# Attention, SoLU layer and experts on one core: gates' chain in two parts, other orders of late rows, query sums and first loads

## The reference

```python
q_pool = q.reshape(B, H, S // 2, 2, D).mean(axis=3)
attn = softmax(q_pool @ k.T / sqrt(D)); x = attn @ v      # to [2304, 512]
h = x @ w_in; solu = h * softmax(h)
x = (solu - mean) / sqrt(var + 1e-6) * g_ln @ w_out
xn = x / (norm(x) + 1e-6); en = emb / (norm(emb) + 1e-6)
logits = xn @ en.T / tau; e = argmax(logits)
gate = softmax(logits)[e]
out = gate * (relu(x @ w1[e]) @ w2[e])
```

## Time and profile before

| | us |
|---|---|
| median of 3 runs | 1046.81 (1045.5 to 1047.55) |
| the profiled execution | 1050.58 |
| its span, first to last instruction | 1048.5 |

### The profile page before, as it was taken

One profiled execution on the slowest core, in us unless ns is written; L12 is line 12 of the kernel. 1 busy time (PEld: TensorE's weight loads), 2 busy tenths in 40 slices (PEclk: granted clock), 3 DMA queues, 4 the chain that ended last, 5 costly groups with the idle time before them and its releaser, 6 DMA issues.

```text
span 1048.5 us, 23488 instructions
## 1 busy us (share of the span) xinstructions
PE 1009.4 (96%) x8143; PEld 716.6 (68%) x8143; DVE 705.3 (67%) x1525; ACT 605.4 (58%) x1356; POOL 386.1 (37%) x438
## 2 busy tenths in 40 slices
PE   8899999999999999989999999988799999999996
PEld 6555555555555555547888888866688888888885
DVE  5778787778887877875599998988746514233111
ACT  5777777878777877754734443363456525333221
POOL 3666555666555564472221222151032111111101
PEclk9999999999999999999999999998899999999999
DMA  4533333333333334125000000054665813311100
GB/s 127 130 89 90 78 82 84 84 75 89 90 80 90 82 74 118 31 83 162 21 21 22 20 31 21 25 189 142 228 213 193 285 51 114 120 42 33 41 22 1
DMA packets 97515, 93.64 MB, mean 89 GB/s; under 512 B 49966, under 2 KB 70446, under 8 KB 97264
## 3 DMA queue, kind: packets, MB, share of 16 engines
q1 hardware_dynamic: 92176, 80.20, 25.7%
q0 software_dynamic: 4000, 11.28, 3.3%
q10 hardware_dynamic: 1216, 0.59, 0.2%
HBM read 74.73 MB, written 11.27 MB: 82 GB/s over the span
## 4 chain that ended last, share of the span: by engine, by line
PE 48%; DVE 2%; issue 1%; ACT 1%; POOL 1%; DMA 1%; DVEq 0%; ACTq 0%; POOLq 0%
PE h_ps L770 9%; PE h_ps L772 9%; PE h_ps L771 9%; PE o_ps L770 5%; PE o_ps L772 5%; PE o_ps L771 5%; PE t_ps L1252 2%; PE t_ps L1142 1%; PE h_ps L1219 1%; DVE junk L1353 1%; DMA w_raw_e<-in_moe_w 1%; PE h_ps L1269 1%; ACT w_split L1752 0%; DVE w_split L1571 0%; PE h_ps L1164 0%
## 5 line engine op out<-in xcount | busy, mean ns | idle before, releaser
L375 POOL TENSOR_SCALAR probs<-probs,raises,recips 128x576 f32<-128x576 f32 x272 | 219.9, 823 | 144.7 <-DVE recips L615 144.7
L588 DVE TENSOR_REDUCE lows<-s_ps 128x1 f32<-128x576 f32 x288 | 205.0, 751 | 73.5 <-PE s_ps L499 71.5
L710 ACT ACTIVATE probs<-s_ps,lows 128x576 f32<-128x576 f32 x272 | 199.0, 736 | 86.6 <-DVE lows L588 85.7
L499 PE MATMUL s_ps<-kt,qt 64*128 64x288 f32 x1024 | 162.3, 433 | 3.2 <-ACT probs L710 1.5
L499 PEld LDWEIGHTS s_ps<-kt,qt 64*128 64x128 f32 x1024 | 87.7, 187 | 106.0 <-ACT probs L710 85.5
L538 PE MATMUL pv_ps<-pt,values 128*64 128x512 f32 x576 | 155.2, 617 | 0.3 <-DVE x_t L637 0.2
L1070 POOL DMA_INDIRECT out<-junk,target_rows x25 | 29.8, 1192 | 261.3 <-ACT junk L1792 261.0
L453 PE MATMUL t_ps<-ident,probs 64*128 64x64 f32 x2178 | 118.6, 226 | 6.8 <-ACT pt L705 4.9
L453 PEld LDWEIGHTS t_ps<-ident,probs 64*128 64x128 f32 x2178 | 107.2, 140 | 20.0 <-DVE pt L622 15.7
L622 DVE COPY pt<-t_ps 128x512 f32<-128x512 f32 x144 | 98.8, 686 | 8.1 <-PE t_ps L453 7.4
L1620 DVE TENSOR_TENSOR y_lo<-t_ps,y_hi 128x512 fp32r<-128x512 f32 x50 | 32.4, 685 | 94.7 <-ACT y_hi L1785 94.7
(11 more groups left out here) (280 smaller groups left out, 2093.5 us busy)
## 6 DMA issues: line engine op xcount, KB each, us to landing
w_raw_e<-in_moe_w SPq DMA_DIRECT2D x60, 512.0 KB, 5.3
k_raw<-in_k SPq DMA_DIRECT2D x32, 256.0 KB, 2.7
q_raw<-in_q SPq DMA_DIRECT2D x30, 256.0 KB, 3.9
qt<-qx SPq DMA_DIRECT2D x60, 128.0 KB, 2.4
token_rows<-x_rows SPq DMA_DIRECT2D x18, 256.0 KB, 2.0
values<-in_v SPq DMA_DIRECT2D x32, 128.0 KB, 2.7
values<-in_v SPq DMA_DIRECT2D x64, 64.0 KB, 2.6
w_raw<-in_moe_w_in SPq DMA_DIRECT2D x4, 512.0 KB, 6.6
```

What stands on the lines that cost most here:

```text
L375: nc.gpsimd.tensor_scalar(where, where, raises[:, par, s, c:c + 1], recips[:, par, s:s + 1], ALU.mult, ALU.mult).then_inc(norm_done if c e ...
L499: last = nc.tensor.matmul(s_ps[c][:, u, 0:part], qt[par][rows(u), s, :], kt[par][rows(u), int(s > full), columns(c)], start=True, stop=True)
L588: nc.vector.tensor_reduce(lows[:, g % 2, s, c:c + 1], s_ps[c][:, :, 0:part], AX.XY, ALU.max, negate=True).then_inc(low_done[c], 1)
L710: nc.scalar.activation(two_halves(probs(g, s)[:])[:, :, columns(c)], s_ps[c][:, :, 0:part], ACT.Exp, bias=lows[:, g % 2, s, c:c + 1], scal ...
```

## The change

VectorE's `weigh` becomes two functions: `shift_logits` (up to the shifted logits) stands where low_first(1) stood, after the steps that give the places of tokens; the rest, still called `weigh`, stands before the loop over tiles, after `split_next(1, ...)`. ScalarE's Exp between them moves from tile 2 to just after `split_next(0, ...)`. low_first(0) moves behind tokens_picked, before low_x(0); low_first(1) behind low_x(1). In tile 1, VectorE and ScalarE do the hidden rows (low_h, high_h) and expert 1's second weights before expert 2's first weights. ScalarE takes the last rows after two of the four weight copies, and copies the turned rows itself (it was VectorE). TensorE does late_dot(1) before the 16 matmuls of the first ids. GpSimd adds the queries of pair g + 2 between the second and third batch of pair g, for every pair; the queries Q and the TAILS of pair 2 are turned in slots 1 and 2 instead of 2 and 3. At the start the second keys are loaded once the first have landed (SP waits), and the second queries once the first have (ScalarE waits).

```diff
--- before.py
+++ after.py
@@ -56,9 +56,8 @@
     FIRST_QA, FIRST_QB = range(4, 6)
-    kq_slots = [{0: KA, 1: Q, 2: TAILS, 7: KB} for at in range(pairs)]
-    kq_slots[0] = {4: KA, 5: Q, 6: TAILS, 7: KB}
-    kq_slots[1] = {0: KA, 2: Q, 3: TAILS, 7: KB}
+    kq_slots = {0: KA, 1: Q, 2: TAILS, 7: KB}
+    first_kq_slots = {4: KA, 5: Q, 6: TAILS, 7: KB}
     rest_slots = (4, 5, 6)
@@ -176,11 +175,11 @@
-            return at + 1 < pairs and s in kq_slots[at]
+            return s in (kq_slots if at else first_kq_slots) and at + 1 < pairs
...
-            return kq_slots[at][s]
+            return (kq_slots if at else first_kq_slots)[s]
@@ -202,7 +201,7 @@
-            return len(kq_slots[0]) * (n - 1) + piece + 1
+            return len(kq_slots) * (n - 1) + piece + 1
@@ -283,6 +282,7 @@
             load_k_tail(0)
+            sp.wait_ge(k_in[0], 16)
             load_b(0)
@@ -380,14 +380,13 @@
             for g in range(pairs):
-                if 1 <= g < pairs - 2:
+                normalise(g, 0)
+                normalise(g, 1)
+                if g + 2 < pairs:
                     add_queries(g + 2)
                     add_tail(g + 2)
-                for b in range(len(batches)):
-                    normalise(g, b)
-                if g == 0:
-                    add_queries(2)
-                    add_tail(2)
+                normalise(g, 2)
+                normalise(g, 3)
             pool.wait_ge(t_done[1], key_tiles * (pairs - 1))
@@ -718,6 +717,7 @@
                 act.dma_start(q_tail[rows(h), :], q_heads[h, main:queries, :]).then_inc(q_tail_in, 16)
+            act.wait_ge(q_in[0], 16)
             load_first_q(1)
@@ -1188,13 +1188,13 @@
             turn_rows(1)
+            late_dot(1)
             for m in range(late):
...
                 nc.tensor.matmul(id_first_ps, row_pick[:, m, :], token_first[:, m, :], start=(m == 0), stop=False)
-            late_dot(1)
             pe.wait_ge(hot_first_ready, 1)
@@ -1479,11 +1479,6 @@
                                     ALU.subtract).then_inc(spots_ready, 1)
-            dve.wait_ge(rows_turned, 2)
-            nc.vector.tensor_copy(x_turned_rows[:, 1, :], turned_rows_ps[1]).then_inc(rows_turned_out, 1)
-
-
-            low_first(0)
             dve.wait_ge(late_dots, 2)
@@ -1533,11 +1528,42 @@
+            def shift_logits():
+
+                dve.wait_ge(powered, 1)
+                refine(inv, inv2, squares)
+                then(nc.vector.tensor_tensor(norms, squares[:, tiles:], inv[:, tiles:], ALU.mult))
+                then(nc.vector.tensor_tensor(norms, norms, inv[:, 0:tiles], ALU.mult))
+                then(nc.vector.tensor_scalar(norms, norms, 1e-6, None, ALU.add))
+                then(nc.vector.reciprocal(norms, norms))
+                then(nc.vector.tensor_tensor(norms, norms, inv[:, 0:tiles], ALU.mult))
+                across = [P, tiles, experts]
+                then(nc.vector.tensor_tensor(work[:], lg[:], row[:].unsqueeze(2).broadcast_to(across), ALU.subtract))
+                nc.vector.tensor_tensor(work[:], work[:], norms.unsqueeze(2).broadcast_to(across),
+                                        ALU.mult).then_inc(shifted, 1)
+
+            def weigh():
+
+                dve.wait_ge(exped, 1)
+                then(nc.vector.tensor_reduce(gates, work[:], AX.X, ALU.add))
+                then(nc.vector.tensor_scalar(gates, gates, 1e-9, None, ALU.add))
+                then(nc.vector.reciprocal(gates, gates))
+                then(nc.vector.tensor_tensor(gates, gates, inv[:, 0:tiles], ALU.mult))
+                then(nc.vector.tensor_copy(gate_parts[:, :, 0], gates))
+                then(nc.vector.tensor_tensor(rest, gates, gate_parts[:, :, 0], ALU.subtract))
+                then(nc.vector.tensor_copy(gate_parts[:, :, 1], rest))
+                then(nc.vector.tensor_tensor(gate_parts[:, :, 2], rest, gate_parts[:, :, 1], ALU.subtract))
+                for i in range(3):
+                    done = nc.vector.tensor_tensor(factor_pick[:, :, :, i], tile_pick[:],
+                                                   gate_parts[:, :, i].unsqueeze(2).broadcast_to(wide), ALU.mult)
+                done.then_inc(factors_picked, 1)
+
             def low_x(t):
...
+            low_first(0)
             low_x(0)
@@ -1565,7 +1591,7 @@
-            low_first(1)
+            shift_logits()
@@ -1587,33 +1613,6 @@
-            def weigh():
...
             def low_h(t):
@@ -1621,6 +1620,7 @@
             low_x(1)
+            low_first(1)
             low_h(0)
@@ -1629,15 +1629,17 @@
             split_next(1, 0, w1_hi_done, w1_lo_done)
+            weigh()
             for t in range(1, slot_tiles):
-                if t == 2:
-                    weigh()
                 if t + 1 < slot_tiles:
                     low_x(t + 1)
+                if t == 1:
+                    low_h(t)
+                    split_next(0, part, w2_hi_done, w2_lo_done)
+                if t + 1 < slot_tiles:
                     split_next(t + 1, 0, w1_hi_done, w1_lo_done)
-                low_h(t)
-                if t == 1:
-                    split_next(0, part, w2_hi_done, w2_lo_done)
+                if t > 1:
+                    low_h(t)
                 if t == 2:
@@ -1733,11 +1735,14 @@
             for c in range(part):
+                if c == part // 2:
+                    rows(last)
+                    act.wait_ge(rows_turned, 2)
+                    nc.scalar.copy(x_turned_rows[:, 1, :], turned_rows_ps[1]).then_inc(rows_turned_out, 1)
+                    square_rows(last)
                 act.wait_ge(first_raw_in[part + c], 16)
...
                 nc.scalar.activation(w_split[:, hi:hi + chunk], w_raw[:, part + c, :], ACT.Copy).then_inc(first_w2_hi, 1)
-            rows(last)
-            square_rows(last)
             act.wait_ge(padded, 1)
@@ -1797,23 +1802,25 @@
             split_next(0, 0, w1_hi_done, up_e_done, 0)
+            act.wait_ge(shifted, 1)
+            nc.scalar.activation(work[:], work[:], ACT.Exp).then_inc(exped, 1)
             act.wait_ge(tiles_known, 1)
...
             for t in range(1, slot_tiles):
-                if t == 2:
-                    act.wait_ge(shifted, 1)
-                    nc.scalar.activation(work[:], work[:], ACT.Exp).then_inc(exped, 1)
                 relu(t)
...
                     high_x(t + 1)
+                if t == 1:
+                    high_h(t)
+                    split_next(0, part, w2_hi_done, down_e_done, 0)
+                if t + 1 < slot_tiles:
                     split_next(t + 1, 0, w1_hi_done, up_e_done, halves * (t + 1))
...
                     scale(t - 1)
-                high_h(t)
+                if t > 1:
+                    high_h(t)
                 if t == slot_tiles - 1:
                     scale(t - 1)
-                if t == 1:
-                    split_next(0, part, w2_hi_done, down_e_done, 0)
                 if t == 2:
```

24 lines of the change are left out of this document (removed).

## The result

The changed kernel takes **1040.0 us** (median of six runs, 1038.74 to 1042.85), the kernel before 1046.7 us beside it (six runs, 1045.5 to 1047.55). The ratio is 0.994, with a 95% interval from 0.9927 to 0.9954: 6.3 us less by the ratio, 6.7 us by the medians. Forecast were 10.9 us. The time lies within the range (1033.0 to 1042.0) but outside the band of 1034 to 1036.9 that had the chance 0.54; some 4 us of the gain are missing.

A forecast was written before the change was run, and what follows sets the result against it. TensorE, busy for 96% of the span, was taken as the bound, with only idle time and 1.2 GHz time to win. 7.1 + 2.2 + 1.6 = 10.9 us off 1046.8 gave 1035.9 us, range 1033.0 to 1042.0.

The forecast's parts named there:

- Gates: Experts, tile 2: splitting VectorE's gates chain removes TensorE's 5.43 us wait and the slow clock behind it; 7.1 us won.
- new stall: Before tile 2's products in the experts: low_x(2) starts later behind the moved chain, so TensorE loses 1.17 us.
- term for the clock: Experts, behind the wait for factor_pick: the 5.8 us stretch at 1.2 GHz goes, taken as 2.8 us won.
- Hand-over: SoLU layer to experts: the row maximum comes 2.5 us sooner, 0.3 us is paid; 2.2 us won, bounds 0.7 and 2.5.
- Second pair: Second pair of heads: earlier query sums and turn slots, without the low clock, win 1.6 us; bounds 0.5 and 2.1.
- Rival 1: Second pair of heads: the clock drops as before, costing 1.1 us, so 1037.0 us; chance 0.18.
- Other pairs: 13 more pairs: GpSimd's sums move to slot 8 at price 0; upper bound 0.45 us a pair, lower -0.3.
- Rival 2: Slot 8 of 13 pairs: GpSimd's additions hold VectorE, TensorE waits 0.45 us each; 5.9 us, 1041.8 us; chance 0.11.
- rival 4: Slots 8 and 0 of 13 pairs: VectorE held at both, 18.2 us lost, so slower at 1054.1 us; chance 0.03.
- First loads: Kernel start: first keys and queries loaded alone win nothing; price 0, between -0.3 and +0.5 us.

The follow-up runs named there:

- after: The changed kernel in its first set of runs, against the kernel before: 1040.0 us, ratio 0.9940.
- e10: The changed kernel with GpSimd's query sum done twice in each pair but the first two: 1048.96 us, 1.0017 of the kernel before.
- before: The kernel without the change, the reference of all ratios: 1046.7 us.
- e2: The kernel before with only GpSimd's new order of sums and normalisations and the second pair's new turn slots: 1046.54 us, 0.9996 of the kernel before.
- e4: The kernel before with only the gates part (VectorE's chain split and moved ahead, with ScalarE's Exp): 1040.16 us, 0.9936 of the kernel before.
- e9: The kernel before with only the hand-over part (late rows, their copy, late_dot, low_first(0)): 1045.62 us, 0.9978 of the kernel before.
- e8: The changed kernel without the two waits that keep the first loads alone: 1038.27 us, 0.9915 of the kernel before.
- after_again: The changed kernel itself, run once more beside the others on the same chip: 1039.27 us, 0.9932 of the kernel before.

## Why the prediction was right and wrong, point by point

**Gates, forecast -7.1: right in the mechanism, 1.3 us too large by the marks.** The wait went, the clock stayed up, factor_pick was early, and ScalarE's copies and SP's loads were in time, as priced. The new stall was given as 1.17 us and measured as 1.17 (13.66 less 12.49). In the profiled pair the stretch G is 6.63 us shorter. Over the three kernels with the old chain G is 33.96, 32.69 and 32.89, a mean of 33.2 against 27.4: the term is 5.8 us in the mean. The difference is the term for the clock. The wait for factor_pick was 5.43, 5.12 and 5.75 us in these three; what is left of the longer turn of tile 3 to that of tile 4 (21.46, 20.19 and 20.40 us against 13.7) is 2.3, 1.4 and 0.9 us for the low clock, 1.5 in the mean. I took 2.8 us, half of a stretch of 5.8, from the one execution that I had, and it was the dearest of three.

**Hand-over, forecast -2.2: right.** In the profiled pair it was 1.24 us at tile 0, which lay within the bounds (0.7), for the reason given there: the fill ran to 713.80 at half rate, 6.75 us instead of 5.64. Over ten kernels with it and 16 matmuls and three without, the turn of tile 0 comes 234.60 against 236.86 us after attention, 2.3 us sooner, the turn of tile 1 1.9 us sooner (242.71 against 244.64), and the part alone took 2.2 us off the median. Some of that is the clock's: in two of the ten (after, e10) and two of the three (before, e2) it is low for 10.2 us here, in the others for 6.8 us or less, and at a like clock the turn of tile 1 is 1.3 to 1.6 us sooner.

**Second pair, forecast -1.6: wrong in sign.** The step that failed stands behind this sentence: "the sum starts when the second batch ends, at 31.1 (...), and is there before slot 1 ends". The sum did so, and the wait for q_sum did go; what the new place costs VectorE in the second pair I put at nothing, without a reason. I moved a GpSimd addition of 1.27 us with one of 0.45 right behind it to beside VectorE's two-input steps of slot 8, and asked what that costs only for the *other* pairs. And there I sized it by the rows at hand, 0.63 us (I wrote 0.62) for a step beside GpSimd's normalisations. These are instructions of 0.8 us each; the additions are longer and follow without a gap, and the step was held through both: 2.34 us. In the second pair VectorE's chain to the probs is what TensorE waits for (it waited 0.58 us for them in the kernel before too), so all of it showed: 2.34 less 0.67 us at `weighted` is 2.25 less 0.58 us at TensorE. The measured term is +1.0 us where the clock stays up in both, and 1.7 to 2.0 where it falls in both. The bound should have been taken from the duration of GpSimd's own instruction. The gain that I had hoped for from the clock was one execution's too: e4 and e9 have the old order and no fall there, so the most to be had from the clock was 0.9 us, and not always.

The Trainium skill (SBUF — State Buffer, section "SBUF: two separate sides") says that VectorE's steps with two inputs in SBUF and GpSimd's instructions that read SBUF exclude each other, each for a whole instruction. The traces agree on the holding, and go further in its length: `weighted` was held from 30.44 over the end of one instruction and the whole of two more, and let go at 32.78. In e10, where a gap of 0.18 us stood between the additions, it was out in the gap. Why it slipped in between q_sum and tail_sum in one case (`low` in e10 ended at 33.69, when q_sum did) and not in the other is not settled.

**Rule of the clock.** In the changed kernel the clock fell at 34.55 us, inside TensorE's wait of 2.25 us for the probs (to 35.03) and before the transposes of the queries (37.25). So the rule of the Trainium skill that the forecast weighed here (TensorE: Matmul & The Clock Gate, "PE-mode transpose": a transpose doesn't count as a busy TensorE) was not put to the test, and no run of this study shows more on it than the start of the trace does. The six executions of the new order have the same transposes there, and the clock fell in two of them. Rival 1, a fall as before, is what these two show, though behind a wait that was longer than before.

**Other pairs, forecast 0: right, with the cover named, though not its thickness.** `weighted` 128x4 went from 149 ns to

```profile
L607 DVE TENSOR_TENSOR weighted<-raises,sums 128x4 f32<-128x4 f32 x13 | 11.8, 909 | 0.0
```

and TensorE's waits for the pt copy stayed at 4.9 us. Rival 2 had the mechanism and the wrong place: the slot 8 of the first pair, not the thirteen others. Doubling the sum showed that 1.27 us more is too much for the cover (0.6 us a pair): the mechanism of rival 4 at slot 8, at about half its price.

**First loads, forecast 0: right**, as far as e8 can tell 1 us.

**Together.** The sum by the marks of all profiled executions is -5.8 (gates) - 1.9 (hand-over) + 1.0 (second pair), so -6.7 us, and the measurement is -6.7. The 4.2 us between forecast and measurement are then 2.6 (second pair), 1.3 (gates, the clock) and 0.3 (hand-over). That the sum meets the measurement to the tenth is luck: it leaves out the falls of the clock in the second pair and the 0.6 us of the later pairs, and after_again gave 7.5 us by the medians. The single parts, timed by themselves, add up to -9.4 us by their ratios (0.9936, 0.9978, 0.9996), 2 to 3 us more than the whole; with intervals of 1 us and more on each I can't say whether that is more than the scatter of the clock's falls.

## What to carry to other kernels

An instruction that moves on GpSimd moves its hold on VectorE with it. List VectorE's steps with two inputs that will then run beside it, price each with the length of the GpSimd instructions that follow one another without a gap, and see first whether VectorE's chain is what TensorE waits for there. Fill GpSimd's idle stretches where VectorE is reducing (`lows`, 751 to 752 ns in the mean in each order of the sums), not where it runs the short steps of a chain. A fall of TensorE's clock that one execution shows is a chance and not a term: look at a second execution before pricing it, and don't shorten filling matmuls without looking at how long TensorE then stands still right behind them.

## What the runs showed of the hardware that I had not expected

- A VectorE step on 4 columns with two inputs took 2.34 us beside GpSimd's back-to-back additions, 0.15 us by itself. With a gap of 0.18 us between two additions it was out in the gap.
- The same program, with the same wait of TensorE (2.25 us) in both executions, had the clock at 1.2 GHz for 6.8 us in one execution (P 26.37) and not at all in another (24.76); the price was 1.6 us.
- The clock had risen under ten matmuls; TensorE then stood still for 2.3 of 3.5 us, and a second low stretch followed (0.62 over 4 us), which took back the 2.6 us won before.
